# Moving each group's weights 64 bytes along SBUF in a kernel whose matmuls run back to back

## The reference

```
sig = 1 / (1 + exp(-f_logit))
f = lower_bound + (1 - lower_bound) * sig
h = f[:, t] * h + (1 - f[:, t]) * x[:, t]     # for each t in turn; y[:, t] = h
x = y.reshape(B * S, 256)                     # 12160 tokens
g = relu(x @ w_in) ** 2                       # w_in 256 x 2048
out = g @ w_out                               # w_out 2048 x 256
```

## Time and profile before

| what | value |
|---|---|
| median of 2 runs | 988.68 us (988.62 to 988.74) |
| the profiled execution | 988.59 us |
| its span, first to last instruction | 986.5 us |
| TensorE matmul busy | 982.4 us (100%), 4388 matmuls |
| VectorE busy | 731.8 us (74%) |
| ScalarE busy | 697.4 us (71%) |
| GpSimd busy | 50.3 us (5%) |
| granted TensorE clock, mean | 1.00 of full speed |

### The profile page before, as it was taken

One profiled execution on the slowest core, in us unless ns is written; L12 is line 12 of the kernel. 1 busy time (PEld: TensorE's weight loads), 2 busy tenths in 40 slices (PEclk: granted clock), 3 DMA queues, 4 the chain that ended last, 5 costly groups with the idle time before them and its releaser, 6 DMA issues.

```text
span 986.5 us, 12612 instructions
## 1 busy us (share of the span) xinstructions
PE 982.4 (100%) x4388; PEld 818.7 (83%) x4388; DVE 731.8 (74%) x940; ACT 697.4 (71%) x925; POOL 50.3 (5%) x50
## 2 busy tenths in 40 slices
PE   9999999999999999999999999999999999999998
PEld 7998888888888888888888888888888888888887
DVE  6997886876877687688688778768768767876545
ACT  8977766766776776676677677677667767766665
POOL 2682000000000000000000000000000000000000
PEclk9999999999999999999999999999999999999999
DMA  9003011002101201100210210110111021001001
GB/s 330 1 15 109 0 44 64 22 1 86 43 1 48 80 0 43 64 21 16 69 43 0 77 51 0 43 64 21 42 43 43 0 85 43 1 1 43 1 1 43
DMA packets 22158, 41.96 MB, mean 43 GB/s; under 512 B 1520, under 2 KB 3056, under 8 KB 22128
## 3 DMA queue, kind: packets, MB, share of 16 engines
q1 hardware_dynamic: 21984, 41.43, 12.1%
q10 hardware_dynamic: 144, 0.13, 0.0%
HBM read 29.11 MB, written 12.45 MB: 42 GB/s over the span
## 4 chain that ended last, share of the span: by engine, by line
PE 100%; DVE 0%; POOL 0%; issue 0%; DVEq 0%; POOLq 0%
PE out_ps L927 52%; PE hidden_ps L912 42%; PE hidden_ps L953 4%; PE out_ps L947 1%; PE out_ps L953 1%; PE out_ps L937 0%; POOL zeros L888 0%; DVE result L848 0%; DVE result L853 0%; DVE result L850 0%; DVEq L852 0%; DVEq L847 0%; POOLq L1204 0%
## 5 line engine op out<-in xcount | busy, mean ns | idle before, releaser
L927 PE MATMUL out_ps<-g_hi,w_out_lo 128*128 128x512 f32 (+1 forms) x760 | 294.2, 387 | 0.0
L927 PE MATMUL out_ps<-g_lo,w_out_hi 128*128 128x512 f32 (+1 forms) x760 | 294.2, 387 | 0.0
L927 PE MATMUL out_ps<-g_hi,w_out_hi 128*128 128x512 f32 (+1 forms) x760 | 294.1, 387 | 0.0
L700 DVE TENSOR_TENSOR g_lo<-h,g_hi 128x1024 fp32r<-128x1024 f32 (+1 forms) x189 | 231.9, 1227 | 64.2 <-ACT g_hi L416 61.0
L409 ACT ACTIVATE h<-h 128x1024 f32<-128x1024 f32 (+1 forms) x189 | 199.2, 1054 | 3.2
L927 PEld LDWEIGHTS out_ps<-g_hi,w_out_hi 128*128 128x128 f32 x760 | 142.7, 188 | 28.3
L927 PEld LDWEIGHTS out_ps<-g_lo,w_out_hi 128*128 128x128 f32 x760 | 142.7, 188 | 28.2
L927 PEld LDWEIGHTS out_ps<-g_hi,w_out_lo 128*128 128x128 f32 x760 | 142.7, 188 | 28.0
L912 PE MATMUL hidden_ps<-sums_hi,wc_hi 128*128 128x512 f32 x352 | 137.0, 389 | 0.0
L912 PE MATMUL hidden_ps<-sums_lo,wc_hi 128*128 128x512 f32 x352 | 137.0, 389 | 0.0
L912 PE MATMUL hidden_ps<-sums_hi,wc_lo 128*128 128x512 f32 x352 | 136.9, 389 | 0.0
(11 more groups left out here) (114 smaller groups left out, 1054.6 us busy)
## 6 DMA issues: line engine op xcount, KB each, us to landing
f_in<-f_logit_t SPq DMA_DIRECT2D x22, 512.0 KB, 4.6
x_in<-x_t SPq DMA_DIRECT2D x22, 512.0 KB, 4.5
out_t<-result SPq DMA_DIRECT2D x20, 512.0 KB, 3.1
w_out_raw<-weights SPq DMA_DIRECT2D x8, 256.0 KB, 6.7
w_in_raw<-weights SPq DMA_DIRECT2D x5, 256.0 KB, 6.5
out_t<-result SPq DMA_DIRECT2D x2, 448.0 KB, 3.0
w_in_raw<-first SPq DMA_DIRECT2D x3, 256.0 KB, 4.1
out_t<-result SPq DMA_DIRECT2D x3, 256.0 KB, 2.0
```

Of the source, the lines that this page charges most:

```text
L700: nc.vector.tensor_tensor(g_lo[b][:, :, 0:n], h_of(it, j, b), g_hi[b][:, :, 0:n].bitcast(F32), ALU.subtract).then_inc(g_ready[b], 1)
L927: mm = nc.tensor.matmul(out_ps[:, b, c, in_bank(it)], half[:, j, m, c * P:(c + 1) * P], moving[b][:, m, 0:n], start=(j == 0 and m == 0 and ...
```

## The change

The four weight tensors become flat, and a helper cuts the groups out of them. Each group takes its blocks and 16 numbers more (`STEP`, 64 bytes), so each group begins 64 bytes further, modulo 512, than the one before. The tensors begin with different groups (`first_place` 0, 1, 3, 4). With the addresses of the compiled program this comes out so: all seven blocks of group `j` in `wc_hi` and `wc_lo`, and the blocks of group `j - 1` in `w_out_hi` and `w_out_lo`, which are used in the same stretch, begin at byte 128 + 64 `j` modulo 512. The padding also shifts what is allocated behind: the moving data now begin at byte 384 instead of 128. So the distance from moving data to weights is 64 (`j` - 4) modulo 512: 256 for group 0, 0 for group 4, 192 for group 7. The tile of zeros is no longer allocated; the zeros lie in the second half of one row of `h1`. No instruction is added, removed or moved, and none changes its size.

```
+STEP = 16
...
-        wc_hi = sb("wc_hi", [P, QUADS, 7, P], F32R)
-        wc_lo = sb("wc_lo", [P, QUADS, 7, P], F32R)
-        w_out_hi = sb("w_out_hi", [P, QUADS, 2, C * P], F32R)
-        w_out_lo = sb("w_out_lo", [P, QUADS, 2, C * P], F32R)
+        def quads_of(name, blocks, m, first_place):
+
+            size = blocks * m + STEP
+            t = sb(name, [P, QUADS * size - STEP], F32R)
+            places = [(first_place + q) % QUADS * size for q in range(QUADS)]
+            return [t[:, k:k + blocks * m].rearrange("p (b m) -> p b m", m=m) for k in places]
+
+
+        wc_hi = quads_of("wc_hi", 7, P, 0)
+        wc_lo = quads_of("wc_lo", 7, P, 1)
+        w_out_hi = quads_of("w_out_hi", 2, C * P, 3)
+        w_out_lo = quads_of("w_out_lo", 2, C * P, 4)
...
         h = [sb(f"h{b}", [P, 2, N]) for b in range(B)]
+
+        zeros = h[1][:, 1, HALF:N].bitcast(mybir.dt.bfloat16)
...
-        zeros = sb("zeros", [P, N], mybir.dt.bfloat16)
...
-                    mm = nc.tensor.matmul(hidden_ps[:, bank, 0:n], half[:, j, w], moving,
+                    mm = nc.tensor.matmul(hidden_ps[:, bank, 0:n], half[j][:, w], moving,
...
-                    mm = nc.tensor.matmul(out_ps[:, b, c, in_bank(it)], half[:, j, m, c * P:(c + 1) * P],
+                    mm = nc.tensor.matmul(out_ps[:, b, c, in_bank(it)], half[j][:, m, c * P:(c + 1) * P],
```

More of the change, by code:

```diff
@@ L391, in plain_w_in_hi @@
                 act.wait_ge(w_in_loaded[q], 16)
-                nc.scalar.copy(wc_hi[:, q, A11:A21 + 1], w_in_raw[:, q]).then_inc(w_plain_hi_done, 1)
+                nc.scalar.copy(wc_hi[q][:, A11:A21 + 1], w_in_raw[:, q]).then_inc(w_plain_hi_done, 1)
             def sum_w_in_hi(q):
@@ L397, in sum_w_in_hi @@
                 act.wait_ge(w_sum_done, 4 * (q + 1))
-                nc.scalar.copy(wc_hi[:, q, S2:S3 + 1], w_in_raw[:, q]).then_inc(w_sum_hi_done, 1)
+                nc.scalar.copy(wc_hi[q][:, S2:S3 + 1], w_in_raw[:, q]).then_inc(w_sum_hi_done, 1)
             def relu_pair1(it, j):
@@ L430, in round_w_out @@
                 act.wait_ge(w_out_loaded[q], 16)
-                nc.scalar.copy(w_out_hi[:, q], w_out_raw[:, q]).then_inc(w_out_hi_done, 1)
+                nc.scalar.copy(w_out_hi[q], w_out_raw[:, q]).then_inc(w_out_hi_done, 1)
             def first_quads():
@@ L658, in first_w_in_lo @@
                 dve.wait_ge(w_plain_hi_done, q + 1)
-                nc.vector.tensor_tensor(wc_lo[:, q, A11:A21 + 1], w_in_raw[:, q],
-                                        wc_hi[:, q, A11:A21 + 1].bitcast(F32), ALU.subtract
+                nc.vector.tensor_tensor(wc_lo[q][:, A11:A21 + 1], w_in_raw[:, q],
+                                        wc_hi[q][:, A11:A21 + 1].bitcast(F32), ALU.subtract
                                         ).then_inc(w_first_ready, 1)
@@ L687, in rest_of_w_out @@
                 dve.wait_ge(w_out_hi_done, q + 1)
-                nc.vector.tensor_tensor(w_out_lo[:, q], w_out_raw[:, q], w_out_hi[:, q].bitcast(F32), ALU.subtract
+                nc.vector.tensor_tensor(w_out_lo[q], w_out_raw[:, q], w_out_hi[q].bitcast(F32), ALU.subtract
                                         ).then_inc(w_out_ready, 1)
@@ L860, in plain_w_in_lo @@
                 pool.wait_ge(w_plain_hi_done, q + 1)
-                nc.gpsimd.tensor_tensor(wc_lo[:, q, A11:A21 + 1], w_in_raw[:, q],
-                                        wc_hi[:, q, A11:A21 + 1].bitcast(F32), ALU.subtract
+                nc.gpsimd.tensor_tensor(wc_lo[q][:, A11:A21 + 1], w_in_raw[:, q],
+                                        wc_hi[q][:, A11:A21 + 1].bitcast(F32), ALU.subtract
                                         ).then_inc(w_plain_ready, 1)
@@ L884, in sum_w_in_lo @@
                 pool.wait_ge(w_sum_hi_done, q + 1)
-                nc.gpsimd.tensor_tensor(wc_lo[:, q, S2:S3 + 1], w_in_raw[:, q],
-                                        wc_hi[:, q, S2:S3 + 1].bitcast(F32), ALU.subtract).then_inc(w_sum_ready, 1)
-            nc.gpsimd.memset(zeros[:], 0.0).then_inc(zeros_done, 1)
+                nc.gpsimd.tensor_tensor(wc_lo[q][:, S2:S3 + 1], w_in_raw[:, q],
+                                        wc_hi[q][:, S2:S3 + 1].bitcast(F32), ALU.subtract).then_inc(w_sum_ready, 1)
+            nc.gpsimd.memset(zeros, 0.0).then_inc(zeros_done, 1)
             plain_w_in_lo(3)
@@ L936, in very_last_second @@
                 for k, (half, moving) in enumerate(((w_out_hi, g_hi), (w_out_hi, g_lo), (w_out_lo, g_hi))):
-                    mm = nc.tensor.matmul(to, half[:, j, m, c * P:(c + 1) * P],
+                    mm = nc.tensor.matmul(to, half[j][:, m, c * P:(c + 1) * P],
                                           moving[b][:, m, columns], start=opens and k == 0,
@@ L946, in warm @@
                 for _ in range(times):
-                    nc.tensor.matmul(out_ps[:, 1, 1], zeros[:, 0:P], zeros[:], start=True, stop=True)
+                    nc.tensor.matmul(out_ps[:, 1, 1], zeros[:, 0:P], zeros, start=True, stop=True)
             def first_part(j, b, c, half, of, opens=False, signal=None, columns=slice(0, NARROW)):
@@ L952, in first_part @@
                 for m, blocks in enumerate(((A11, A12), (A21, A22))):
-                    mm = nc.tensor.matmul(banks[:, m, columns], half[:, j, blocks[c]],
+                    mm = nc.tensor.matmul(banks[:, m, columns], half[j][:, blocks[c]],
                                           first_block(*of, b, c)[:, columns], start=opens, stop=signal is not None,
```

## The result

The changed kernel takes 1003.36 us (two runs, 1003.31 to 1003.40) against 988.68 us: a ratio of 1.0148 with a 95% interval from 1.0105 to 1.0192. It is slower by 14.7 us. The forecast of 989.6 us was not met; the time lies inside the range, within the 2% that the prediction called no change, and beside the 1005 us of the rival called "no rhythm".

A forecast was written before the change was run, and what follows sets the result against it. TensorE's back-to-back matmuls were taken to bound the kernel. 3936 matmuls x 0 plus 0.9 us for seams, on the profiled 988.59 us, gave 989.5, and 0.1 more for the median 989.6 us; range 966 to 1007 us.

The forecast's parts named there:

- no rhythm: Rival, matmul steps: streams stay out of step at seven of eight distances, 4.8 ns each, 16.5 us, 1005 us; chance 0.21.
- What bounds the kernel: Whole kernel: TensorE, busy 982.4 of 986.5 us, sets the end by how fast matmuls follow one another, 226.7 ns.
- rounding and splitting, the zeros: Weight preparation on ScalarE, VectorE and GpSimd, and zeros moved into `h1`: hidden beside TensorE, cost 0.
- the one on the distance: Matmul steps within groups: new distance from moving data to weights adds zero; bounds 9.7 ns less to 8 ns more.
- the fourth row: Last 256-column matmuls: first surplus read as 3 to 7 ns, half or less of 13.3, so mostly in the streaming itself.
- The rows that spoke of a loss: Trace before, 448-to-512-column change and last group after short gaps: steps of 230 to 231.5 ns when out of step.
- The seam term: Boundaries between groups: finding the rhythm anew costs 0.02 us at each of 87 seams, 1.7 us at most; half taken, 0.9.
- The faster rival: Matmul steps: the aligned case was the bad one; other distances free 6.7 ns each, 23 us, 966 us; chance 0.17.

The follow-up runs named there:

- all64: Changed kernel with weights packed as before the change and weights and moving data alike 64 bytes later, distance 0 in all groups: 988.9 us.
- bf16_reads: Changed kernel, same placement, from iteration 0's second products on reading only the upper 16 bits of each fp32 number as bf16 at 4-byte stride: 983.74 us.
- bf16_packed: Changed kernel with packed layout of before; from iteration 0's second products on, bf16 zeros as weights and packed bf16 data, 2 bytes a column: 944.4 us.
- data64: Changed kernel with weights exactly where they were before the change and only the moving data 64 bytes later, distance 192 modulo 256 in all groups: 996.47 us.
- one_seam: Changed kernel with distance 192 modulo 256 in every group except group 3, which has 176: 1004.98 us in four runs, ratio 1.0162.

## Why the prediction missed its point and kept its range

**What bounds the kernel** was right: the changed time is the number of matmuls by the step, and everything else hides. The other terms put at zero (rounding and splitting, the zeros) were zero: all64 has the new home of the zeros and shifted addresses without the new distances, and is at the old time.

**The step that failed** is the one on the distance: "I take zero for the steady step, as it is nearest to the fourth row, and because nothing in the trace ties the surplus to an address." Measured are +6.4, +5.7 and +2.4 ns at 64, 128 and 192, and 0 at 256: a mean of 15.0 us / 3960 = 3.8 ns. The fourth row, was also misread. Only the first step of 256 columns has a surplus of 3 to 7 ns; the nine behind it take 0.120 us each, 13.3 ns over their 106.7, as much as with 512 columns. So the row doesn't show a surplus that halves with the columns. What it was used for, that the old step is near a floor, was borne out by the runs all the same (nothing that kept the 4-byte stream and full fp32 went below it at 512 columns, and bf16_reads took 1 ns off). But a floor says that nothing is to be gained. It says nothing of what can be lost, and I used it against both. The rows that spoke of a loss, and the earlier trace rows, showed the same instructions at 230 to 232 ns when out of step, and they were the nearest rows for a kernel that is put out of step.

**The rival "no rhythm"** named the cause, that the good rhythm doesn't hold at other distances, and nearly the size: 4.8 ns at seven of eight distances, 1005 us, measured 1003.4. It was wrong in two details. One of the seven, 256, is free, since the pattern repeats every 256 bytes. And the other groups don't fail to settle: they settle into other rhythms that cost more. The argument against it, "timing is free to settle at other distances too", was true and no comfort. That its 4.8 ns is also the mean price of the six groups that pay, (6.4 + 5.7 + 2.4) / 3, is luck: they lie between 2.4 and 6.4.

**The range** held because it took in the middle of this rival, and with some luck. Groups 3 and 7 ran near 229.1 ns at distance 192, where other kernels had 233.3. As an estimate, 22 groups x 45 x 4.2 ns = 4.2 us more would have made it 1007.5, just outside, and no row of before could say which of the two rhythms would come.

**The seam term** had the right price, 0.02 us where a group at distance 0 is entered; but there are 22 such seams and not 87, so 0.4 us for the 0.9 taken. At the other seams the search can't be told from the group's own price.

**The faster rival** fell: no distance of the 22 tried, in steps of 16 bytes and of 4 below 32, went under 226.7 ns with 512 columns; with 448 the distance of 192 did gain, 2.7 ns, which no term of the prediction had. Of the two rules of the Trainium skill, "TensorE: Matmul & The Clock Gate", "Back-to-back issue gap", gives 215.8 ns for 512 columns; bf16_packed, at 215.7, agrees, and the fp32 stream of this kernel does not. "SBUF — State Buffer", "Who interferes with whom", has two independent read ports of a TensorE that never waits; data64, where the distance alone adds 2.2 ns a step, speaks against it.

**What stays open.** Why the pattern has a period of 256 bytes, why 0 and 16 share the good rhythm and 4 doesn't, and what picks one of two rhythms, was not settled, nor why 192 is worse than 0 with 512 columns and better with 448; the runs show that it is so and that the load beside the stream takes part. All variants but one_seam were run once; the kernel before, over all its runs, lies between 988.48 and 989.28 us. Distances finer than 16 bytes were tried only below 32, nor different distances for the three matmuls of a product.

## What to carry to other kernels

When TensorE runs without a gap, read the distance between the starts of its matmuls and compare it by stage: a kernel can lose 1.5% with no new wait in its profile. With matmuls of 512 columns, keep the fp32 weights and the fp32 data that stream beside their loads at one distance of 0 modulo 256 bytes for the whole kernel; pads that broke this cost 0.7 to 2.1% here and can change the rhythm of what comes behind them too. With another number of columns measure it anew: with 448, 192 was better than 0. And when a row shows that a quantity is at its floor, lower only the chance of a gain.

## What was not expected of the hardware

- Back-to-back fp32 matmuls of 512 columns have steady rhythms, 226.7 ns at best (distances 0 and 16 modulo 256 bytes of data and weights) and 228.4 to 234.9 at the others; 4 bytes are enough to leave the best one.
- At one distance (192) 228.9 and 233.3 ns are both steady, each for seven groups of 45 matmuls on end, and a stretch of 45 matmuls at another distance switches between them. Distance 16 showed both 226.7 and 233.3.
- With 448 columns the order is the other way: 202.7 ns at distance 0, 200.0 at 192.
- Weight loads of 64 columns instead of 128 made the step at distance 0 longer, 229.8 ns.
- With 4 bytes a column in stream and load, 512 columns cost 225.6 ns even in bf16; with both packed they take 215.7.
